# Eight plain products in the second pair too, and more identity products ahead of the first data

## The chip, the cores and the metric

The program runs on one core of a Trainium2 chip. The metric is the device time in microseconds (us) of one execution; less is better. TensorE is called PE here, VectorE DVE, ScalarE ACT, GpSimd POOL, and SyncE SP, as in the profile.

## The reference

```python
kv = np.einsum('bhsd,bhse->bhde', k, v)          # batch 4, heads 8, seq 576, head dim 64
out = np.einsum('bhsd,bhde->bhse', q, kv)
rms = np.sqrt(np.mean(out * out, axis=-1, keepdims=True) + 1e-06)
x = out / rms * g_norm                            # then heads side by side: x is 2304 x 512
h = x @ w_in                                      # 512 x 2048
x = (h * (1.0 / (1.0 + np.exp(-h)))) @ w_out      # 2048 x 512
y = ((x @ w_a) * (x @ w_b)) @ w_out2              # 512 x 1536 twice, 1536 x 512
```

All of it is float32.

## The kernel before

The tokens are worked on in two groups of 1152 (two batches each). Group 0's attention stands first, alone; then come four segments: layer 1 of group 0, layer 1 of group 1, layer 2 of group 0, layer 2 of group 1. Group 1's attention is cut into small slots (`attend(at)`) that stand between the matmuls of layer 1.

A segment runs over **pairs**: a pair is 256 columns of the up weights. For a pair the kernel needs a 2 x 2 block product, (two halves of the 512 features) x (two halves of the tokens), and forms it from seven products instead of eight, by Strassen's method in Winograd's form: POOL makes sums of weight quarters, and once in a segment DVE and POOL make sums of the x quarters (s1 to s4, in `x_sums`). To keep float32 accuracy each operand is split in a high and a low part (`x_hi`, `x_lo`; `w_hi`, `w_lo`), and each product is 12 matmuls of 128x128 by 128x288 (hi*hi, hi*lo, lo*hi; two halves c of the contraction; two halves s of the tokens). A product of seven adds results: ACT copies a partial sum (`part`, into `kept`), DVE adds it (`add`). Then ACT makes the sigmoid, DVE multiplies (`silu`), ACT rounds g to its high part (`g_round`), DVE makes the low part (`g_rest`). For a plain product x itself is the operand, and no sum of x or of weights is wanted.

The **first pair** already uses eight plain products (table `PLAIN`, function `plain(k)` on PE, line 750), since the sums of x are not there yet. It is short of other work: its down products stand in the second pair. In the first pair of before DVE and POOL also make the sums of x for the second pair and split them: on DVE `half_sum` (line 1275), `last_sum` (1283) and `half_rest` (1290), on POOL `half_sum` (567) and `half_rest` (574). Operands are numbered: 0, 3, 6, 7 are quarters of x, 1, 2, 4, 5 are the sums. The **second pair** then uses the seven products in an order of its own (`SECOND_STEPS`), and between them stand the 16 down tiles of the first pair, 6 matmuls each (`down1`, lines 798 to 800), which DVE takes out of PSUM (`flush1`, line 1370) from two banks that the tiles and the attention slots use in turn.

Each engine has its own list of instructions, in the order in which the code calls them, and waits on semaphores: PE waits for `w_ready` (weights split by POOL into a ring of four), `x_ready` and `side_ready` (x split by DVE and POOL), `g_ready` (a result bank read out to the end), and `flushed`. The order is written out by hand in the functions `first_pair`, `second_pair` and `layer1` of each engine.

At the very start PE multiplies the identity by itself `WARM` = 9 times (line 898), then turns q of head pair 0 (`q_turn`, line 679), and then waits for k and v by DMA (`kv`, line 665; its eviction is `kv_keep` on ACT; `q_kv`, line 691, follows it; `o_turn`, line 701, turns the result).

Of the kernel before, what the change touches and what calls it, by code (L numbers as in the profile page):

```python
# [11 lines left out]
P = 128  # L12
# [3 lines left out]
def fused_attention_ffn_kernel(nc, q, k, v, g_norm, w_in, w_out, w_a, w_b, w_out2, out):  # L16
# [51 lines left out]
    FIRST_TILES = (0, 3, 1, 2)  # L68
    FIRST_ENDS = {0: 3, 3: 4, 1: 5, 2: 7}
    FIRST_BANK = {0: BANK_A, 1: BANK_C, 2: BANK_A, 3: BANK_B}  # L70

    SECOND_STEPS = (5, 3, 0, 1, 2, 4, 6)
# [4 lines left out]
    DVE_RESTS = (((3, 0), (6, 0), (3, 1), (6, 1), (2, 0), (2, 1), (1, 0), (1, 1), (4, 0), (4, 1)),  # L77
# [5 lines left out]
    WARM = 9  # L83

    with ExitStack() as ctx:
# [139 lines left out]
        def at_step(u, n):  # L225

            return SECOND_STEPS.index(n) if u == 1 else n

        def after(u, n):

            return len(PLAIN) + STEPS * (u - 1) + at_step(u, n) + 1

        def weight(u, n):

            return RING + STEPS * (u - 1) + at_step(u, n)

        def sums_before(u, per):

            return per * (u - 1)

        def g_count(pp, tile):

            return 4 * pp + (FIRST_TILES.index(tile) if pp == 0 else tile) + 1

        def place(pp, tile):
            if pp == 0:
                return both(FIRST_BANK[tile])
            return halves(held[:, 2, :]) if tile == 2 else both({0: BANK_B, 1: BANK_A, 3: BANK_C}[tile])
# [61 lines left out]
        for pp in range(PAIR0[-1] + 1):  # L310
            tiles = D_TILES[SEGS[seg_of(pp - 1)][1]] if pp else 0
            steps = STEPS if pp < PAIR0[1] else 0
            for n in range(steps):
                slot_turn.append(turns)
                at = STEPS * pp + n
                turns += SLOT_BANKS[at % SLOTS] if at < SLOTS * PAIRS else 0
                for _ in range(TILES_AFTER[n] if pp else 0):
                    tile_turn.append(turns)
                    turns += 1
# [23 lines left out]
        def x_summed(seg, n, c=1):  # L343

            if seg == 0:
                if n == 5:
                    return side_sum, c + 1
                at = {1: 1, 2: 2, 4: 3}[n]
                return (x_sum, at) if c else (side_sum, 2 + at)
# [14 lines left out]
        def temps(seg):  # L364

            if seg == 0:
                return [x_sums[:, n] for n in (2, 1, 4, 5)]
# [18 lines left out]
        def _(sp):  # L386
            def raw_free(r):
# [6 lines left out]
                elif r == 0:  # L394
                    sp.wait_ge(w_ready, RING)
# [66 lines left out]
        def _(pool):  # L462
# [6 lines left out]
            def ready(u, step, src):  # L469
                n = weight(u, step)  # L470

                pool.wait_ge(prod, (3, 5, 7, 8)[n - RING] if n < 2 * RING else n + 1)
# [42 lines left out]
            def second_up():  # L515
                b11, b12, b21, b22 = quarters(1)
                nc.gpsimd.tensor_tensor(t2, b22, b12, ALU.subtract).then_inc(w_sum, 1)
                pool.wait_ge(w_sum, 1)
                ready(1, 5, t2)
                ready(1, 3, b21)  # L520
                nc.gpsimd.tensor_tensor(t0, b12, b11, ALU.subtract).then_inc(w_sum, 1)
                ready(1, 0, b11)
                pool.wait_ge(w_sum, 2)
                nc.gpsimd.tensor_tensor(t1, b22, t0, ALU.subtract).then_inc(w_sum, 1)
                pool.wait_ge(w_sum, 3)
                ready(1, 1, t1)
                ready(1, 2, t0)
                ready(1, 4, b22)
                pool.wait_ge(w_ready, weight(1, 2) + 1)
                nc.gpsimd.tensor_tensor(t0, b21, t1, ALU.subtract).then_inc(w_sum, 1)  # L530
                pool.wait_ge(w_sum, 4)
                ready(1, 6, t0)

            def head_pairs():
# [103 lines left out]
            second_up()  # L638
            lower(1)
# [6 lines left out]
        def _(pe):  # L646
# [91 lines left out]

            def plain(k):

                n, w, bank, begins = PLAIN[k]
                pe.wait_ge(w_ready, w + 1)
                at = PLAIN_SLOT[w]
                for c in range(2):
                    pe.wait_ge(*x_split(0, n, c))
                    hi, lo = w_hi[:, at, c, :], w_lo[:, at, c, :]
                    for w_part, x, first, last in ((hi, x_hi, c == 0, False), (hi, x_lo, False, False),
                                                   (lo, x_hi, False, c == 1)):
                        for s in range(2):
                            mm = pe.matmul(ps[:, bank + s, 0:PART], w_part,  # L750
                                           x[:, x_place(n), c, s * PART:(s + 1) * PART],
                                           start=(begins and first), stop=last, skip_group_check=not begins)
                mm.then_inc(prod, 1)

            def may_begin(u, n):
# [4 lines left out]
                if u == 1 and n in (1, 2, 4, 5):  # L760
# [4 lines left out]
                if n in STEP_BEGINS:  # L765
# [6 lines left out]
                    else:  # L772
                        tile = ({0: 2, 3: 3, 5: 1} if pp == 1 else {0: 1, 3: 0, 5: 3})[n]
# [12 lines left out]
            def down1(pp, n):  # L786
# [4 lines left out]
                pe.wait_ge(g_ready, g_count(pp, (1, 2)[m] if pp == 0 else 2 * m + 1))  # L791
# [54 lines left out]

            def layer1(pp):
# [759 lines left out]
```

## Time and profile before

| | |
|---|---|
| median of 3 runs | 897.32 us (896.08 to 897.57) |
| profiled execution | 897.5 us, of which the span of the profile is 895.7 |
| PE busy | 868.0 us (97%) |
| weight loads of PE (PEld) | 821.9 us (92%) |
| DVE, ACT, POOL busy | 520.8, 282.0, 626.3 us |

PE is nearly always busy after the start, so the share of PE's idle time by stretch, and the places where it waits, are what there is to read. "PEclk" is the clock that the throttle granted.

### The profile page before, as it was taken

To read this page: it belongs to the slowest core of one execution; us is meant where nothing else is said; L and a number is where in the kernel's file an instruction comes from. 1 tells how busy PE (TensorE), PEld (TensorE's weight loads), DVE (VectorE), ACT (ScalarE), POOL (GpSimd) and SP (SyncE) were. 2 spreads that over 40 slices of the span, in tenths; PEclk is the share of its full clock that TensorE was granted. 3 is DMA by queue.
4 is the path that set the end of the run, shared out by engine and by line. 5 is a ranking of instruction groups with operands and counts; after the bars stand their busy time and mean duration, and the time that the engine had idled before them with its cause. 6 is when DMAs were issued, how large, how long until landed. Compare 5 with 4: busy or idle time off the path is not lost.

```text
span 895.7 us, 16996 instructions
## 1 busy us (share of the span) xinstructions
PE 868.0 (97%) x6582; PEld 821.9 (92%) x6582; DVE 520.8 (58%) x816; ACT 282.0 (31%) x470; POOL 626.3 (70%) x911
## 2 busy tenths in 40 slices
PE   7889999999999999999999999999999999999998
PEld 6678899999999999999989999999998999999996
DVE  2697575657887665556774454453573544545536
ACT  2764353434543322222432121121251221211210
POOL 1596446654597777775588687887979877777760
PEclk9999999999999999999999999999999999999999
DMA  9742232510011111111111011111110250111103
GB/s 269 177 101 75 67 62 56 120 47 26 27 45 48 48 49 48 49 48 48 33 40 48 25 48 50 46 48 48 48 48 25 84 140 24 52 48 44 48 25 106
DMA packets 47103, 55.63 MB, mean 62 GB/s; under 512 B 11952, under 2 KB 32432, under 8 KB 47024
## 3 DMA queue, kind: packets, MB, share of 16 engines
q1 hardware_dynamic: 44304, 49.55, 20.1%
q10 hardware_dynamic: 2720, 4.98, 1.9%
q8 instruction: 54, 0.88, 0.4%
q14 instruction: 25, 0.20, 0.1%
HBM read 49.81 MB, written 4.72 MB: 61 GB/s over the span
## 4 chain that ended last, share of the span: by engine, by line
PE 86%; DVE 7%; POOL 2%; issue 2%; ACT 1%; DMA 1%; SPq 0%; DVEq 0%; ACTq 0%; POOLq 0%
PE ps L734 45%; PE ps L798 7%; PE ps L799 7%; PE ps L800 7%; PE ps L820 5%; PE ps L822 5%; PE ps L821 5%; PE ps L691 2%; DVE x_lo L1290 2%; DMA kvq<-in_v_dram 1%; PE ps L665 1%; PE ps L701 1%; DVE g_lo L1358 1%; DVE o_sb L1249 1%; DVE ps L1336 1%
## 5 line engine op out<-in xcount | busy, mean ns | idle before, releaser
L734 PE MATMUL ps<-x_hi,w_hi 128*128 128x288 f32 x1092 | 236.5, 298 | 4.8 <-ACT kept L1038 2.4
L734 PE MATMUL ps<-x_lo,w_hi 128*128 128x288 f32 x1092 | 234.0, 296 | 0.0
L734 PE MATMUL ps<-x_hi,w_lo 128*128 128x288 f32 x1092 | 232.9, 295 | 0.0
L734 PEld LDWEIGHTS ps<-x_hi,w_hi 128*128 128x128 f32 x1092 | 179.1, 188 | 17.1 <-POOL w_lo L478 5.0
L734 PEld LDWEIGHTS ps<-x_hi,w_lo 128*128 128x128 f32 x1092 | 176.1, 189 | 0.0
L734 PEld LDWEIGHTS ps<-x_lo,w_hi 128*128 128x128 f32 x1092 | 174.7, 188 | 0.0
L476 POOL TENSOR_SCALAR w_hi<-wt 128x256 fp32r<-128x256 f32 x156 | 70.4, 451 | 129.4 <-PE ps L734 125.1
L798 PE MATMUL ps<-g_hi,d_hi 128*128 128x288 f32 x512 | 154.2, 301 | 3.2 <-DVE g_lo L1358 1.2
L1038 ACT COPY kept<-ps 128x576 f32<-128x576 f32 x117 | 75.1, 642 | 254.2 <-PE ps L734 253.4
L1372 DVE TENSOR_TENSOR xy<-xy,ps 128x288 f32<-128x288 f32 x224 | 100.8, 453 | 88.5 <-PE ps L800 87.5
L800 PE MATMUL ps<-g_hi,d_lo 128*128 128x288 f32 x512 | 150.9, 295 | 0.0
L799 PE MATMUL ps<-g_lo,d_hi 128*128 128x288 f32 x512 | 150.9, 295 | 0.0
L478 POOL TENSOR_TENSOR w_lo<-wt,w_hi 128x256 fp32r<-128x256 f32 x156 | 117.6, 754 | 13.0
L1382 DVE TENSOR_TENSOR xy<-xy,ps 128x512 f32<-128x512 f32 x90 | 61.6, 685 | 95.1 <-PE ps L822 95.1
L798 PEld LDWEIGHTS ps<-g_hi,d_hi 128*128 128x128 f32 x512 | 96.4, 188 | 6.9 <-issue 3.2
L478 POOL TENSOR_TENSOR w_lo<-raw,w_hi 128x256 fp32r<-128x256 f32 x121 | 90.1, 745 | 10.1
L476 POOL TENSOR_SCALAR w_hi<-raw 128x256 fp32r<-128x256 f32 x121 | 51.4, 425 | 65.1 <-PE ps L734 65.1
L800 PEld LDWEIGHTS ps<-g_hi,d_lo 128*128 128x128 f32 x512 | 96.1, 188 | 0.0
L799 PEld LDWEIGHTS ps<-g_lo,d_hi 128*128 128x128 f32 x512 | 96.1, 188 | 0.0
L1063 ACT CAST g_hi<-ps 128x576 fp32r<-128x576 f32 x85 | 54.5, 642 | 102.7 <-DVE ps L1347 52.2
L820 PE MATMUL ps<-d_hi,g_hi 128*128 128x512 f32 x216 | 85.2, 395 | 0.0
L822 PE MATMUL ps<-d_hi,g_lo 128*128 128x512 f32 x216 | 84.7, 392 | 0.0
(104 smaller groups left out, 1211.4 us busy)
## 6 DMA issues: line engine op xcount, KB each, us to landing
raw<-in_moe_w_out_dram SPq DMA_DIRECT2D x28, 512.0 KB, 3.8
raw<-in_moe_w_in_dram SPq DMA_DIRECT2D x15, 512.0 KB, 3.5
raw<-in_moe_w_a_dram SPq DMA_DIRECT2D x12, 512.0 KB, 3.6
raw<-in_moe_w_b_dram SPq DMA_DIRECT2D x12, 512.0 KB, 3.5
kvq<-in_k_dram SPq DMA_DIRECT2D x12, 288.0 KB, 5.1
kvq<-in_v_dram SPq DMA_DIRECT2D x12, 288.0 KB, 6.6
out_dram<-xy SPq DMA_DIRECT2D x27, 128.0 KB, 2.4
kvq<-in_q_dram SPq DMA_DIRECT2D x16, 144.0 KB, 6.4
```

What stands on the lines that cost most here:

```text
L476: nc.gpsimd.tensor_scalar(w_hi[:, slot], src, 1.0, 0.0, ALU.mult, ALU.add).then_inc(w_high, 1)
L478: nc.gpsimd.tensor_tensor(w_lo[:, slot], src, w_hi[:, slot].bitcast(F32), ALU.subtract).then_inc(w_ready, 1)
L734: mm = pe.matmul(ps[:, bank + s, 0:PART], w, x[:, n, c, s * PART:(s + 1) * PART], start=(begins and first), stop=last, skip_group_check=no ...
L798: pe.matmul(dst, hi, g_hi[:, f, part], start=(f == 0), stop=False)
L799: pe.matmul(dst, hi, g_lo[:, f, part], start=False, stop=False)
L800: mm = pe.matmul(dst, lo, g_hi[:, f, part], start=False, stop=(f == 1))
L820: pe.matmul(dst, hi, d_hi[:, pp % 2, f, :], start=(f == 0), stop=False)
L822: mm = pe.matmul(dst, lo, d_hi[:, pp % 2, f, :], start=False, stop=(f == 1))
L1038: nc.scalar.copy(halves(kept[:, n, :]), both(BANK_A)).then_inc(part_kept, 1)
L1063: nc.scalar.copy(halves(g_at_half(g_hi, pp, m, f)), src).then_inc(g_high, 1)
L1372: nc.vector.tensor_tensor(dst, dst, src, ALU.add).then_inc(flushed, 1)
L1382: nc.vector.tensor_tensor(dst, dst, src, ALU.add).then_inc(flushed, 1)
```

## The change

The second pair is given eight plain products too, from the same quarters of x, and the same weight quarters of its own columns. So POOL makes four weight splits for it instead of four sums and seven splits, ACT no partial copies and DVE no adds. The sums of x and their splits, which stood in the first pair, are made in the second pair (operand 4's split in the third), for the third pair, which is now the first with seven products. `lower(0)` (the split of the first down weights) stands on POOL ahead of the sums of x. The sum s4 gets a place of its own, in `held`. At the start PE has 12 identity products ahead of the turns of q and 13 more behind them, instead of 9 and none.

```diff
-    PLAIN = ((0, 0, BANK_A, True), (0, 1, BANK_C, True), (7, 0, BANK_B, True), (3, 2, BANK_A, False),
-             (6, 2, BANK_B, False), (3, 3, BANK_C, False), (7, 1, BANK_A, True), (6, 3, BANK_A, False))
+    PLAIN = (((0, 0, BANK_A, True), (0, 1, BANK_C, True), (7, 0, BANK_B, True), (3, 2, BANK_A, False),
+              (6, 2, BANK_B, False), (3, 3, BANK_C, False), (7, 1, BANK_A, True), (6, 3, BANK_A, False)),
+             ((0, 0, BANK_B, True), (3, 2, BANK_B, False), (0, 1, BANK_C, True), (3, 3, BANK_C, False),
+              (7, 0, BANK_A, True), (6, 2, BANK_A, False), (7, 1, BANK_B, True), (6, 3, BANK_B, False)))
-    SECOND_STEPS = (5, 3, 0, 1, 2, 4, 6)
+    PLAIN_PAIRS = 2
+    PLAIN_TILES_AFTER = 2
-    WARM = 9
+    WARM = (12, 13)
...
@@ POOL
             def second_up():
-                ...            (four sums of weight quarters, seven splits)
+                quarter = quarters(1)
+                def second_split(at):
+                    w = PLAIN_SLOT.index(at)
+                    pool.wait_ge(prod, after(0, max(k for k in range(8) if PLAIN[0][k][1] == w)))
+                    split(RING + at, at, quarter[w])
+                second_split(0)
+                second_split(1)
+                half_sum(5, 0)
+                half_sum(5, 1)
+                second_split(2)
+                second_split(3)
+                half_sum(1, 0)
+                half_sum(2, 0)
             def head_pairs():
...
-                half_sum(5, 0)
-                half_sum(5, 1)
-                half_sum(1, 0)
-                half_sum(2, 0)
-                half_rest(5, 0)
-                half_rest(5, 1)
             head_pairs()
             lower(0)
             second_up()
+            half_rest(5, 0)
+            half_rest(5, 1)
             lower(1)
@@ PE
+            def second_pair():
+                t = 0
+                for k in range(len(PLAIN[1])):
+                    if PLAIN[1][k][3]:
+                        pe.wait_ge(g_ready, (g_count(0, 3), g_count(0, 1), g_count(0, 2), g_count(1, 0))[k // 2])
+                    plain_half(1, k, 0)
+                    if k < STEPS:
+                        attend(STEPS + k)
+                    plain_half(1, k, 1)
+                    for _ in range(PLAIN_TILES_AFTER):
+                        down1(0, t)
+                        t += 1
-            for _ in range(WARM):
-                pe.matmul(ps[:, BANK_D, 0:P], ident[:], ident[:], start=True, stop=True)
+            warm(WARM[0])
             for j in range(JS):
                 q_turn(0, 0, j, first_bank(0, j))
+            warm(WARM[1])
             kv(0, 0)
@@ ACT
             def first_pair():
...
-                first_round(5)
-                first_round(1)
                 sigmoid(0, 0)
                 attend(1, True)
-                first_round(2)
                 g_round(0, 0)
...
             def second_pair():
+                at = STEPS
+                attend(at, False)
+                sigmoid(1, 0)
+                attend(at + 2, True)
+                first_round(5)
+                g_round(1, 0)
+                attend(at + 3, True)
+                first_round(1)
+                sigmoid(1, 1)
+                attend(at + 4, True)
+                g_round(1, 1)
+                first_round(2)
+                attend(at + 5, True)
...
@@ DVE
             def first_pair():
...
                 half_rest(3, 1)
-                half_sum(1)
                 half_rest(6, 1)
-                half_sum(2)
                 silu(0, 0)
-                half_rest(2, 0)
                 g_rest(0, 0)
...
             def second_pair():
+                half_sum(1)
                 flush(0, 1)
                 norm(at + 1)
-                flush(2, 4)
+                flush(2, 3)
+                last_sum()
                 norm(at + 2)
+                silu(1, 0)
...
```

On PE, at the start of the program, the list is this before (`ident` is the identity, `q_tiles` are q's tiles, `kvq` holds k and v of a head pair):

```order
L898 MATMUL ps<-ident 128x128 x9
L679 MATMUL ps<-ident,q_tiles_53 128x128 x9
L665 MATMUL ps<-kvq_71 64x64 x36
L691 MATMUL ps<-kv_sb,qT_sb 64x128 x18
L665 MATMUL ps<-kvq_72 64x64 x36
L679 MATMUL ps<-ident,q_tiles_54 128x128 x9
```

and this in the change:

```order
L917 MATMUL ps<-ident 128x128 x12
L678 MATMUL ps<-ident,q_tiles_53 128x128 x9
L917 MATMUL ps<-ident 128x128 x13
L664 MATMUL ps<-kvq_71 64x64 x36
L690 MATMUL ps<-kv_sb,qT_sb 64x128 x18
L664 MATMUL ps<-kvq_72 64x64 x36
L678 MATMUL ps<-ident,q_tiles_54 128x128 x9
```

Thirteen products stand between the turns of q and the first product of k and v.

On DVE, in the first pair, from the last normalised tiles of the attention on, before:

```order
L1249 TENSOR_TENSOR o_sb<-ps,stat 128x384 x3
L1290 TENSOR_TENSOR x_lo<-xy,x_hi 128x576 x3
L1275 TENSOR_TENSOR x_sums<-xy,x_sums 128x576
L1290 TENSOR_TENSOR x_lo<-xy,x_hi 128x576
L1275 TENSOR_TENSOR x_sums<-xy 128x576
L1336 TENSOR_TENSOR ps<-held,ps 128x2x288
L1290 TENSOR_TENSOR x_lo<-x_sums,x_hi 128x576
L1358 TENSOR_TENSOR g_lo<-ps,g_hi 128x576
```

and in the change:

```order
L1268 TENSOR_TENSOR o_sb<-ps,stat 128x384 x3
L1308 TENSOR_TENSOR x_lo<-xy,x_hi 128x576 x4
L1354 TENSOR_TENSOR ps<-held,ps 128x2x288
L1376 TENSOR_TENSOR g_lo<-ps,g_hi 128x576
L1354 TENSOR_TENSOR ps<-held,ps 128x2x288
```

The two sums (`x_sums`) and the split of a sum are gone from between x's splits and the first `silu` and `g_rest`.

On DVE again, in the second pair of the change, from the first sum on, the flushes are the `COPY xy<-ps` rows:

```order
L1294 TENSOR_TENSOR x_sums<-xy,x_sums 128x576
L1388 COPY xy<-ps 128x288 x2
L1254 RECIPROCAL stat<-stat 128x18
L1268 TENSOR_TENSOR o_sb<-o_sb,stat 128x384
L1388 COPY xy<-ps 128x288 x2
L1301 TENSOR_TENSOR held<-xy,x_sums 128x1152
L1268 TENSOR_TENSOR o_sb<-o_sb,stat 128x384
L1354 TENSOR_TENSOR ps<-held,ps 128x2x288
L1388 COPY xy<-ps 128x288 x2
L1376 TENSOR_TENSOR g_lo<-ps,g_hi 128x576
L1294 TENSOR_TENSOR x_sums<-xy 128x576
```

The sums now stand between the flushes of the down tiles.

## Rows read from the trace of the kernel before

**Rows 1.** The page: busy time (share, instructions); and one group, its mean in ns.

```profile
PE 868.0 (97%) x6582; PEld 821.9 (92%) x6582; DVE 520.8 (58%) x816; ACT 282.0 (31%) x470; POOL 626.3 (70%) x911
...
L1063 ACT CAST g_hi<-ps 128x576 fp32r<-128x576 f32 x85 | 54.5, 642 | 102.7 <-DVE ps L1347 52.2
```

**Rows 2.** Busy time by stretch: us, then PE, PEld, DVE, ACT, POOL, clock, DMA share, GB/s.

```profile
65.50:96.00 30.50, 28.22 (x268) 26.61 (x265) 22.30 (x35) 13.65 (x25) 18.95 (x26) 1.00 0.27 65
```

**Rows 3.** Timeline of PE, 0 to 27 us: start, duration, what, count [idle before, releaser].

```profile
1.56 4.21 PE L898 MATMUL ps<-ident 128*128 128x128 f32 x18 [1.56 <-POOL ident L466]
6.86 2.18 PE L679 MATMUL ps<-ident,q_tiles 128*128 128x128 f32 x9 [1.09 <-POOL q_tiles L582]
11.91 2.20 PE L665 MATMUL ps<-kvq 64*64 64x64 f32 x72 [2.86 <-DMA kvq<-in_v_dram]
15.13 4.11 PE L691 MATMUL ps<-kv_sb,qT_sb 128*64 128x128 f32 x36 [1.02 <-issue]
19.16 2.09 PE L665 MATMUL ps<-kvq 64*64 64x64 f32 x72
21.18 1.20 PE L679 MATMUL ps<-ident,q_tiles 128*128 128x128 f32 x9
...
23.39 0.88 PE L691 MATMUL ps<-kv_sb,qT_sb 128*64 128x128 f32 x12
...
26.76 1.28 PE L665 MATMUL ps<-kvq 64*64 64x64 f32 x72
```

**Rows 4.** Timeline of POOL, the copies of q's tiles of head pairs 0 to 2.

```profile
6.30 1.40 POOL L582 COPY q_tiles<-kvq 128x384 f32<-128x384 f32 x3 [4.79 <-DMA kvq<-in_q_dram]
18.09 1.41 POOL L582 COPY q_tiles<-kvq 128x384 f32<-128x384 f32 x3 [10.39 <-DMA kvq<-in_q_dram]
24.26 1.41 POOL L582 COPY q_tiles<-kvq 128x384 f32<-128x384 f32 x3 [4.76 <-DMA kvq<-in_q_dram]
```

**Rows 5.** Timeline of PE in the first pair and at its end.

```profile
52.23 0.43 PE L750 MATMUL ps<-x_hi,w_lo 128*128 128x288 f32 x2
54.27 0.53 PE L750 MATMUL ps<-x_hi,w_hi 128*128 128x288 f32 x2 [1.60 <-DVE x_lo L1290]
...
57.09 0.49 PE L679 MATMUL ps<-ident,kvq 128*128 128x128 f32 x3
59.75 0.53 PE L750 MATMUL ps<-x_hi,w_hi 128*128 128x288 f32 x2 [2.17 <-DVE g_lo L1358]
...
65.57 0.53 PE L734 MATMUL ps<-x_hi,w_hi 128*128 128x288 f32 x2
```

**Rows 6.** Timeline of DVE in the first pair, and one later split of x.

```profile
44.62 5.81 DVE L1290 TENSOR_TENSOR x_lo<-xy,x_hi 128x576 fp32r<-128x576 f32 x3
...
54.13 1.98 DVE L1275 TENSOR_TENSOR x_sums<-xy 128x576 f32<-128x576 f32 x1
...
57.34 1.69 DVE L1290 TENSOR_TENSOR x_lo<-x_sums,x_hi 128x576 fp32r<-128x576 f32 x1 [0.55 <-ACT x_hi L1025]
...
75.85 0.75 DVE L1290 TENSOR_TENSOR x_lo<-x_sums,x_hi 128x576 fp32r<-128x576 f32 x1
```

**Rows 7.** Timeline of POOL, the first sums of x, and the second pair.

```profile
44.59 3.32 POOL L567 TENSOR_TENSOR x_sums<-xy 128x576 f32<-128x576 f32 x2
...
77.07 0.41 POOL L476 TENSOR_SCALAR w_hi<-wt 128x256 fp32r<-128x256 f32 x1 [3.05 <-PE ps L734]
```

**Rows 8.** Groups of DVE by form, 65.5 to 96.1 us: count, busy us, mean ns, idle before.

```profile
L1370 DVE COPY xy<-ps 128x288 f32<-128x288 f32 x14 | 6.0, 451 | 4.2 <-PE ps L800 4.2
L1290 DVE TENSOR_TENSOR x_lo<-x_sums,x_hi 128x576 fp32r<-128x576 f32 x4 | 4.6, 1179 | 0.0
...
L1336 DVE TENSOR_TENSOR ps<-held,ps 128x576 f32<-128x576 f32 x3 | 2.3, 755 | 0.4 <-ACT held L1050 0.4
L1283 DVE TENSOR_TENSOR x_sums<-xy,x_sums 128x1152 f32<-128x1152 f32 x1 | 1.8, 1791 | 0.0
```

**Rows 9.** Timeline of PE, the first matmuls of the third pair.

```profile
96.04 0.42 PE L734 MATMUL ps<-x_hi,w_hi 128*128 128x288 f32 x2
```

More of the change, by code:

```diff
@@ L315, in fused_attention_ffn_kernel @@
                 at = STEPS * pp + n
-                turns += SLOT_BANKS[at % SLOTS] if at < SLOTS * PAIRS else 0
-                for _ in range(TILES_AFTER[n] if pp else 0):
+                turns += SLOT_BANKS[at % SLOTS] if n < STEPS and at < SLOTS * PAIRS else 0
+                for _ in range(0 if pp == 0 else PLAIN_TILES_AFTER if pp == 1 else TILES_AFTER[n]):
                     tile_turn.append(turns)
@@ L393, in raw_free @@
                     sp.wait_ge(d_ready, 2 * (PAIR0[n] + p + 1))
-                elif r == 0:
-                    sp.wait_ge(w_ready, RING)
+                elif p < PLAIN_PAIRS and n == 0:
+                    sp.wait_ge(w_ready, RING * (p + 1))
                 else:
@@ L737, in half, with plain_half @@
                     mm.then_inc(prod, 1)
-            def plain(k):
[L741 to L753, printed above, removed]
+            def plain_half(pp, k, c):
+                n, w, bank, begins = PLAIN[pp][k]
+                at = PLAIN_SLOT[w]
+                if c == 0:
+                    pe.wait_ge(w_ready, w + 1 if pp == 0 else RING + at + 1)
+                if pp == 0:
+                    pe.wait_ge(*x_split(0, n, c))
+                hi, lo = w_hi[:, at, c, :], w_lo[:, at, c, :]
+                for w_part, x, first, last in ((hi, x_hi, c == 0, False), (hi, x_lo, False, False),
+                                               (lo, x_hi, False, c == 1)):
+                    for s in range(2):
+                        mm = pe.matmul(ps[:, bank + s, 0:PART], w_part,
+                                       x[:, x_place(n), c, s * PART:(s + 1) * PART],
+                                       start=(begins and first), stop=last, skip_group_check=not begins)
+                if c == 1:
+                    mm.then_inc(prod, 1)
+            def plain(k):
+                plain_half(0, k, 0)
+                plain_half(0, k, 1)
             def may_begin(u, n):
@@ L894, in layer2, with warm @@
                 down2(pp - 1, 8)
+            def warm(count):
+                for _ in range(count):
+                    pe.matmul(ps[:, BANK_D, 0:P], ident[:], ident[:], start=True, stop=True)
             pe.wait_ge(consts, 3)
-            for _ in range(WARM):
-                pe.matmul(ps[:, BANK_D, 0:P], ident[:], ident[:], start=True, stop=True)
+            warm(WARM[0])
             for j in range(JS):
                 q_turn(0, 0, j, first_bank(0, j))
+            warm(WARM[1])
             kv(0, 0)
@@ L919, in _ @@
             first_pair()
-            for pp in range(1, PAIR0[-1]):
+            second_pair()
+            for pp in range(PLAIN_PAIRS, PAIR0[-1]):
                 if SEGS[seg_of(pp)][1] == 1:
@@ L1022, in first_round @@
                 if n == 4:
-                    act.wait_ge(prod, 7)
+                    act.wait_ge(prod, after(1, 6))
                 nc.scalar.copy(x_hi[:, n], operand(0, n)).then_inc(x_high, 1)
@@ L1041, in sigmoid @@
                 u, idx = prods_of(pp)[0], g_count(pp, tile) - 1
-                if pp == 0:
-                    act.wait_ge(prod, FIRST_ENDS[tile] + 1)
+                if pp < PLAIN_PAIRS:
+                    act.wait_ge(prod, after(pp, PLAIN_ENDS[pp][tile]))
                 elif tile == 1:
@@ L1414, in flush @@
                         flush1(0, n)
+                half_sum(1)
                 flush(0, 1)
                 norm(at + 1)
-                flush(2, 4)
+                flush(2, 3)
+                last_sum()
                 norm(at + 2)
-                half_rest(4, 0)
-                flush(5, 7)
+                silu(1, 0)
+                dve.wait_ge(*x_summed(0, 4))
+                flush(4, 5)
+                g_rest(1, 0)
+                half_sum(2)
                 norm(at + 3)
-                half_rest(4, 1)
-                add(u, 0, both(BANK_B))
+                flush(6, 7)
+                silu(1, 1)
+                dve.wait_ge(*x_summed(0, 2, 0))
+                dve.wait_ge(*x_summed(0, 2))
                 flush(8, 9)
-                add(u, 1, halves(held[:, 2, :]))
+                g_rest(1, 1)
+                half_rest(1, 0)
                 flush(10, 11)
-                silu(1, 0)
-                g_rest(1, 0)
+                half_rest(1, 1)
+                silu(1, 3)
                 flush(12, 13)
-                silu(1, 1)
-                g_rest(1, 1)
+                g_rest(1, 3)
+                half_rest(2, 0)
+                flush(14, 15)
                 silu(1, 2)
-                add(u, 2, both(BANK_C))
-                flush(14, 15)
+                half_rest(2, 1)
                 g_rest(1, 2)
-                silu(1, 3)
-                g_rest(1, 3)
             def layer1(pp):
@@ L1452, in layer1 @@
                 late_rest(pp, 0)
+                if pp == 2:
+                    half_rest(4, 0)
                 if pp == 7:
@@ L1458, in layer1 @@
                 late_rest(pp, 1)
+                if pp == 2:
+                    half_rest(4, 1)
                 next_rest(pp, 0)
```

98 lines of the change are left out of this document (31 added, 67 removed).

## The prediction

> **What bounds the kernel now.** I read the page first. PE is busy 868.0 of 895.7 us [rows 1], so what can be won is the rest, and any product added costs its full time unless it fills a hole. So I asked for PE's timeline and looked for places where its starts stand further apart than its matmuls need. They lie almost all in the first 100 us, in three parts.
>
> *The start.* PE multiplies the identity until 5.8 us, waits for q's tiles, turns them, and then stands from 9 to 11.9 us waiting for v by DMA [rows 3]. The reader is to see that the same work costs two prices there: nine turns take 2.18 us at 6.86 and 1.20 us at 21.18; 72 records of k and v take 2.20 us at 11.91, 2.09 us at 19.16, and 1.28 us at 26.76; twelve records of `q_kv` take 0.88 us at 23.39, and 36 take 4.11 us at 15.13 [rows 3]. That is PE's lower level, 1.2 GHz, up to about 21.1 us, and 2.4 GHz from there on. The column of the granted clock doesn't show it (it reads 1.00 in every stretch I asked for); the distances do: eight gaps between nine turns, less one tail, are (2.18 - 0.42)/8 = 0.22 us and later (1.20 - 0.15)/8 = 0.13 us. Ahead of the rise PE had worked without a real pause from 15.13 us, 6 us; the identity products of before are one stretch of 3.9 us, after which it stood 1.1 us.
>
> *The first pair.* PE's starts at 52.23 and 54.27 are two matmuls (0.27 us) apart by count, so 1.77 us are lost, to DVE's `x_lo`. Three turns from 57.09 need 0.35 us, and the next start is 59.75: 2.31 us lost, to `g_lo` [rows 5]. Both come from DVE's list [rows 6]: three splits of x take 5.81 us together, a sum 1.98 us, a split 1.69 us, while later one split of the same shape takes 0.75 us. In the slow stretch POOL is working on x as well (two sums in 3.32 us [rows 7]).
>
> *The second pair.* From 65.57 [rows 5] to 96.04 [rows 9] are 30.47 us. A step of product is 12 matmuls, and six issues of two stand 0.265 us apart, 1.59 us; seven are 11.1 us. A down tile is 6 matmuls, 0.79 us; 16 are 12.7. The slots of the attention in it (three `o_turn` at a third of a us, one `kv` at 1.28 less its tail, one `q_turn`) come to 2.5 us. That is 26.3 us, so 4.2 us are lost. By busy time it is less, 30.50 - 28.22 = 2.3 us [rows 2], since the ends are modelled and cover part of each hole; I go by starts.
>
> **The change, part by part.**
>
> *Identity products.* 12 are 24 records at 0.22 us (18 took 4.21 us, less a tail of 0.42, over 17 gaps [rows 3]), 5.3 us, from 1.56 to 6.85. The turns of q could start at 6.86 before, POOL's copy being the limit (6.30 us [rows 4]), and still can: this part costs nothing, and its cover is that copy; without it it would cost 1.3 us (six records more). Then 13 more, 26 records: at the lower level 5.6 us, from 8.7 to 14.3, which is 2.4 us past the arrival of v at 11.9; at the upper level half, 2.8 us, done at 11.5 and hidden by that DMA. Which holds is decided by whether the clock is up by then. Now PE works from 1.56 on without a pause over 0.2 us, 7 us by the time the 13 begin, and 6 us was what stood ahead of the rise before. I take it that the clock is up. The Trainium skill (TensorE: Matmul & The Clock Gate, Part 1) says that the throttled state is the default and activity releases it; the prices above agree.
>
> Then `kv` takes 0.8 us less (2.09 against 1.28), `q_kv` of head 0 takes 3 x 0.81 = 2.4 us instead of 4.03: PE would be at the second `kv` at 16.75 instead of 19.16, and through it at 18.0. But q of head pair 1 lands at 18.09, and PE follows the copy by 0.56 us (6.30 to 6.86 [rows 3, 4]): its turns start at 18.65 instead of 21.18. That is 2.5 us, and the DMA caps it. The next, 24.26 + 0.56 = 24.8, is before PE's shifted time (about 25.4), so nothing takes it back. ACT, DVE and POOL follow PE in this part. **Term: -2.5 us**; bounds: 0 (clock not up, where the 2.4 us of delay are about paid back by the work behind it at full clock), and -2.9.
>
> *First pair.* DVE has the fourth split of x right behind the third. POOL works on `lower(0)` beside it, so I leave the slow price: 44.62 + 4 x 1.94 = 52.4 us at the latest, where PE asks at 52.5. So the 1.77 us go. `silu(0,0)` follows at once (0.76), `g_round` on ACT takes 0.64 [rows 1, 8], `g_rest` 0.76: with hand-overs of 0.1 us, ready at 54.6 to 54.9. PE comes there after two products less the hole, at 55.5. The 2.31 us go too, with 0.6 us to spare. What is late next would be `g_rest(0, 1)`, behind ACT's square of the first `q_kv`; by the same prices it is done near 59.7, and its tile is wanted at 62.8. **Term: -4.1 us**; bounds -3.2 and -4.3 (with the slower first matmul after each wait).
>
> *Second pair.* One product more: **+1.6 us**, on PE's own time, hidden by nothing. Three `part`, three `add`, four weight sums and three weight splits less; those were off the path (POOL stood 3.05 us waiting for PE at one split alone [rows 7]). The four splits of the second pair wait for the first pair's products 3, 5, 7 and 8 and are done some 0.5 to 7 us before they are wanted. What can cost is DVE: its list now has sums and splits between the flushes, and a flush that is late holds one of two banks, and so PE. Its work there: 16 flushes at 0.45, four `silu` and four `g_rest` at 0.76, six halves of x at 1.18, one whole sum 1.79, three normalised tiles at about 1.0 (a SBUF-only form like `x_lo`, two thirds as long): 7.2 + 6.1 + 7.1 + 1.8 + 3.0 = 25.2 us [rows 8], in 27.9 us of PE's work. Stepping through the list by these prices I get waits of about 0.3 us at the third turn, 0.5 us at the tile behind `kv` (it waits for ACT's eviction, before as now), and a few tenths at the end; I take 1.5 us for what I can't place, so the 4.2 become 1.5: **-2.7 us**. Bounds: 0.7 left, and all 4.2 left.
>
> The Trainium skill (SBUF — State Buffer, SBUF: two separate sides) speaks against this part: the port pair of DVE and POOL is an exclusive lock for a DVE operation with two SBUF inputs against a POOL operation that reads SBUF, and the loser waits for the whole instruction. The trace agrees: 1.94 us in the slow stretch, 0.75 us with POOL idle. By that rule alone, each of the six halves in the second pair would be at 1.98 us, and DVE's work at 30.0 us, more than PE's 27.9. It would hold only if POOL were always busy.
>
> *Third pair.* It takes `half_rest(4, c)`, and ACT's rounding of operand 4 (1.2 us) ahead of an eviction that PE's bank waits for. It had waits of the same size at this place. I count 0, bounds 0 and +1.0. Everything behind is PE's own pace as before.
>
> **Sum.** -2.5 - 4.1 + 1.6 - 2.7 = -7.7 us. The profiled execution is 897.5 us (895.7 and 1.8 around it), 0.2 us from the median of 897.3, so 889.8 from the one and 889.6 from the other; I say 889.6.
>
> **The rivals.**
>
> *The clock isn't up, or the 13 products run past 11.9 us.* For it: where the clock rose before, real data was being multiplied; half of the new stretch is turns. Then the first term is 0: 892.1, and 891 to 893.5. Chance 0.19.
>
> *DVE is the bound of the second pair.* DVE's work at the slow price is 30.0 us, with the restarts about 31: the second pair lasts 31 instead of my 29.4, and 0.5 us more in the third: 891.7. Against: POOL waits for PE in much of it. Chance 0.13.
>
> *Slower.* The ten operations of DVE on SBUF alone (six halves, one whole sum, three normalised tiles) each hold a flush. Two banks give a flush 0.79 us before PE stands, so an operation of 1.98 us can cost 1.2 us; ten are 12 us. Then the second pair is 27.9 + 12 = 39.9 us against 30.5, +9.4, and with -6.6 of the other terms the kernel ends at 900.1. It decides from about 0.9 us each (8.4 us in all, for +1.8). Against: in the second pair of before four splits and one whole sum stood between the flushes too [rows 8], and all its waits together were 4.2 us. Chance 0.04.
>
> *The work is only moved.* All that the first pair gains is paid back in the third, which now wants the sums: 897.3 - 2.5 + 1.6 = 896.4. Against: the sums have 25 us more. Chance 0.03.
>
> *Better:* all holes go and the kernel is under 887.5. Chance 0.07. **The forecast** has 0.54, in 887.6 to 891.2.
>
> **The numbers.** A measurement tells 0.2% (1.8 us) from no change. Faster: 0.54 + 0.19 + 0.13 + 0.07 = 0.93; same 0.03; slower 0.04. The range leaves out the slower case, the moved case and the edges of the others: 887.0 to 893.2.
>
> **What would show it.** In the profile after: turns of q at 6.86 and nine of them in 1.2 to 2.2 us; the 13 products end before 11.9 us; `q_kv` 36 records in about 2.5 us; the second head's turns at 18.65. No wait for `x_lo` or `g_lo` over 0.3 us in the first pair; second pair begins near 59.0 and ends near 88.4, with PE's waits for `xy` (flush) as the sign of DVE's part. The prediction is wrong if the 13 products are over 0.4 us each, or if DVE has no idle time in the second pair.

## The result, and the profile after

The changed kernel takes 895.09 us (median of 20 runs, 893.36 to 896.98), the kernel before 897.79 us on the same chips (20 runs, 895.17 to 899.60). The ratio is 0.9974, with a 95% interval from 0.9965 to 0.9984: faster by 2.7 us, or 0.3%, where 7.7 us were forecast. The profiled execution is 895.0 us (span 893.2), against 897.5 us (span 895.7) before. Three stretches tell the story: up to the third pair, from there to 240 us, and around 674 us.

**Up to the third pair** the kernel did more than was forecast. The timeline of PE at the start answers to [rows 3]:

```profile
1.57 4.65 PE L917 MATMUL ps<-ident 128*128 128x128 f32 x24 [1.57 <-POOL ident L469]
6.75 1.45 PE L678 MATMUL ps<-ident,q_tiles 128*128 128x128 f32 x9 [0.53 <-POOL q_tiles L579]
8.03 3.07 PE L917 MATMUL ps<-ident 128*128 128x128 f32 x26
11.63 1.28 PE L664 MATMUL ps<-kvq 64*64 64x64 f32 x72 [0.53 <-DMA kvq<-in_v_dram]
13.94 2.19 PE L690 MATMUL ps<-kv_sb,qT_sb 128*64 128x128 f32 x36 [1.03 <-issue]
...
18.55 0.50 PE L664 MATMUL ps<-kvq 64*64 64x64 f32 x18 [1.32 <-issue]
19.11 1.45 PE L678 MATMUL ps<-ident,q_tiles 128*128 128x128 f32 x9
...
38.28 0.53 PE L750 MATMUL ps<-x_hi,w_hi 128*128 128x288 f32 x2
...
58.13 0.53 PE L750 MATMUL ps<-x_hi,w_hi 128*128 128x288 f32 x2
...
86.81 0.42 PE L733 MATMUL ps<-x_hi,w_hi 128*128 128x288 f32 x2
```

The 13 products behind the turns end at 11.1 us, ahead of v at 11.63, and `kv` takes 1.28 us and `q_kv` 2.19, both the upper level's prices, where before they took 2.20 and 4.11. The last three rows are the first plain product of the first pair, the start of the second pair, and the start of the third. They stood at 41.35, 65.57 [rows 5] and 96.04 [rows 9] before. So PE leads by 3.07, 7.44 and 9.23 us, and the second pair takes 28.68 us instead of 30.47.

POOL's copy of q for the second head pair, which answers to the second of [rows 4], is held by the DMA:

```profile
18.55 1.41 POOL L579 COPY q_tiles<-kvq 128x384 f32<-128x384 f32 x3 [10.96 <-DMA kvq<-in_q_dram]
```

The timeline of DVE, which answers to [rows 6]:

```profile
41.55 1.96 DVE L1308 TENSOR_TENSOR x_lo<-xy,x_hi 128x576 fp32r<-128x576 f32 x2
44.06 2.90 DVE L1308 TENSOR_TENSOR x_lo<-xy,x_hi 128x576 fp32r<-128x576 f32 x2 [0.54 <-ACT x_hi L1039]
...
50.61 0.76 DVE L1376 TENSOR_TENSOR g_lo<-ps,g_hi 128x576 fp32r<-128x576 f32 x1 [0.70 <-ACT g_hi L1087]
```

All four splits of x are done at 46.96 us, and the first `g_lo` at 51.37, where PE asks for it at 52.33. PE waits for neither any more. In the second pair DVE's operations by form are these (count, busy us, mean ns, idle before):

```profile
L1388 DVE COPY xy<-ps 128x288 f32<-128x288 f32 x15 | 6.7, 454 | 7.5 <-PE ps L805 7.5
...
L1376 DVE TENSOR_TENSOR g_lo<-ps,g_hi 128x576 fp32r<-128x576 f32 x4 | 3.0, 750 | 0.4 <-ACT g_hi L1087 0.4
L1308 DVE TENSOR_TENSOR x_lo<-x_sums,x_hi 128x576 fp32r<-128x576 f32 x3 | 2.5, 827 | 0.0
```

The flushes wait 7.5 us for PE's tiles, and in PE's waits of this pair none is for a flush: DVE is never the later one. Three of the splits have a mean of 827 ns, where [rows 8] had 1179.

**From the third pair to about 240 us** the lead melts. Here is the same work in both: a stretch of the kernel before (first fence), and one that holds nearly the same instructions after (second). The columns are those of [rows 2].

```profile
98.00:240.00 142.00, 139.30 (x1210) 134.26 (x1209) 89.41 (x162) 61.39 (x108) 77.59 (x115) 1.00 0.26 63
```

```profile
89.00:236.00 147.00, 142.63 (x1207) 134.24 (x1206) 90.90 (x162) 61.90 (x109) 77.70 (x116) 1.00 0.25 61
58.10:86.80 28.70, 28.61 (x278) 28.06 (x277) 20.63 (x35) 15.06 (x25) 17.20 (x19) 1.00 0.38 85
```

1210 and 1207 matmuls, 134.2 us of weight loads in both, a granted clock of 1.00 in both, and yet 5.0 us more. The second row of the second fence is the second pair, where PE is busy 28.61 of 28.70 us. By PE's starts the lead is still 9.1 us at the first turn of the fourth pair (127.47 us before, 118.33 after). From there it shrinks by a few tenths at a time to 4.3 us at the tile behind the last attention slot (239.35 and 235.09), and then it stays. What PE waits for in the longer stretch is seen in the chain of its weight loads and its matmuls (total us, times, longest). Before:

```profile
PE ps L798 <- ACT qT_sb L978: 0.6, 1, 0.6
...
PEld ps L798 <- issue: 1.4, 3, 0.8
```

After:

```profile
PE ps L803 <- ACT qT_sb L1002: 1.1, 2, 0.7
PE ps L803 <- ACT xy L982: 0.5, 1, 0.5
PE ps L803 <- ACT o_sb L969: 0.2, 1, 0.2
...
PEld ps L803 <- issue: 4.5, 15, 0.7
```

L803 is the first matmul of a down tile, and what it waits for on ACT are evictions of the attention: turned q (`qT_sb`), the output (`o_sb`), and the output turned (`xy`). Fifteen times a weight load of a down tile comes late, against three before. The profile names nothing that these wait for ("issue"); that the banks are behind them too is shown by e1 and e2 below. One such place, PE's timeline before:

```profile
148.16 0.49 PE L679 MATMUL ps<-ident,kvq 128*128 128x128 f32 x3
...
149.01 0.43 PE L734 MATMUL ps<-x_hi,w_lo 128*128 128x288 f32 x2
149.28 0.29 PE L798 MATMUL ps<-g_hi,d_hi 128*128 128x288 f32 x1
```

and after:

```profile
139.26 0.52 PE L678 MATMUL ps<-ident,kvq 128*128 128x128 f32 x3
...
140.15 0.43 PE L733 MATMUL ps<-x_hi,w_lo 128*128 128x288 f32 x2
140.98 0.37 PE L803 MATMUL ps<-g_hi,d_hi 128*128 128x288 f32 x1 [0.41 <-ACT qT_sb L1002]
```

The order is the same: a turn of q, half a product, a down tile. The tile now stands 0.83 us behind the last start instead of 0.27, because it waits for the turn's eviction. A tile has to wait for the eviction of the turn just ahead of it only if both use one bank.

**Around 674 us** the last loss stands, of another kind. The timeline of PE after:

```profile
673.93 0.65 PE L733 MATMUL ps<-x_hi,w_hi 128*128 128x288 f32 x2 [1.89 <-POOL w_lo L481]
674.38 0.68 PE L733 MATMUL ps<-x_lo,w_hi 128*128 128x288 f32 x2
...
677.26 0.59 PE L733 MATMUL ps<-x_lo,w_hi 128*128 128x288 f32 x2
677.68 0.42 PE L733 MATMUL ps<-x_hi,w_lo 128*128 128x288 f32 x2
```

the row of its stretch, where the third number from the end is the granted clock:

```profile
675.00:680.00 5.00, 5.00 (x27) 4.79 (x26) 0.76 (x1) 0.64 (x1) 4.75 (x9) 0.74 0.30 100
```

and the timeline of the same place before:

```profile
678.13 0.53 PE L734 MATMUL ps<-x_hi,w_hi 128*128 128x288 f32 x2 [1.87 <-POOL w_lo L478]
```

Both kernels stand 1.9 us there, for POOL's split of a weight at the first pair of the last segment. In this execution of the changed kernel the granted clock went down behind it (0.74 as a mean of 675 to 680 us, the issues of two matmuls 0.48 us apart instead of 0.265, which is 1.2 against 2.4 GHz). Eight distances from 673.93 to 677.68 are 3.75 us instead of 2.1, so 1.6 us are lost.

The three add up: 9.2 us of lead at the third pair, less 5.0, less 1.6, is 2.6; the spans differ by 2.5.

### The profile page after: what moved, and what is told of

Same layout as the page of the kernel before. It is cut to its first block, busy times and chain, and to the rows that moved or that the text cites. A ratio compares the mean times of both kernels' runs of the same rounds, so it can differ in the third digit from the quotient of the medians.

```text
span 893.2 us, 17059 instructions
## 1 busy us (share of the span) xinstructions
PE 872.3 (98%) x6626; PEld 824.4 (92%) x6626; DVE 512.3 (57%) x813; ACT 279.9 (31%) x467; POOL 618.0 (69%) x901
## 4 chain that ended last, share of the span: by engine, by line
PE 89%; DVE 4%; POOL 2%; issue 2%; DMA 1%; ACT 1%; SPq 1%; DVEq 0%; ACTq 0%; POOLq 0%
PE ps L733 44%; PE ps L803 8%; PE ps L805 7%; PE ps L804 7%; PE ps L825 5%; PE ps L827 5%; PE ps L826 5%; PE ps L750 3%; PE ps L690 2%; DMA kvq<-in_q_dram 1%; PE ps L700 1%; PE ps L664 1%; POOL w_lo L481 1%; PE ps L678 1%; DVE ps L1354 0%
## 5 line engine op out<-in xcount | busy, mean ns | idle before, releaser
L733 PE MATMUL ps<-x_hi,w_hi 128*128 128x288 f32 x1064 | 230.5, 298 | 5.0 <-ACT kept L1062 2.3
L733 PE MATMUL ps<-x_lo,w_hi 128*128 128x288 f32 x1064 | 228.7, 297 | 0.0
L733 PE MATMUL ps<-x_hi,w_lo 128*128 128x288 f32 x1064 | 227.4, 295 | 0.0
L733 PEld LDWEIGHTS ps<-x_hi,w_hi 128*128 128x128 f32 x1064 | 175.2, 189 | 17.2 <-issue 5.0
L733 PEld LDWEIGHTS ps<-x_hi,w_lo 128*128 128x128 f32 x1064 | 172.2, 189 | 0.0
L733 PEld LDWEIGHTS ps<-x_lo,w_hi 128*128 128x128 f32 x1064 | 171.0, 189 | 0.0
L803 PE MATMUL ps<-g_hi,d_hi 128*128 128x288 f32 x512 | 155.1, 303 | 2.9 <-ACT qT_sb L1002 1.1
L1062 ACT COPY kept<-ps 128x576 f32<-128x576 f32 x114 | 73.2, 642 | 253.0 <-PE ps L733 252.2
L481 POOL TENSOR_TENSOR w_lo<-wt,w_hi 128x256 fp32r<-128x256 f32 x152 | 114.1, 751 | 12.7
L803 PEld LDWEIGHTS ps<-g_hi,d_hi 128*128 128x128 f32 x512 | 96.4, 188 | 8.5 <-issue 5.8
L805 PEld LDWEIGHTS ps<-g_hi,d_lo 128*128 128x128 f32 x512 | 96.1, 188 | 0.0
L804 PEld LDWEIGHTS ps<-g_lo,d_hi 128*128 128x128 f32 x512 | 96.1, 188 | 0.0
```

Source lines behind the costliest of these rows:

```text
L481: nc.gpsimd.tensor_tensor(w_lo[:, slot], src, w_hi[:, slot].bitcast(F32), ALU.subtract).then_inc(w_ready, 1)
L733: mm = pe.matmul(ps[:, bank + s, 0:PART], w, x[:, n, c, s * PART:(s + 1) * PART], start=(begins and first), stop=last, skip_group_check=no ...
L803: pe.matmul(dst, hi, g_hi[:, f, part], start=(f == 0), stop=False)
L804: pe.matmul(dst, hi, g_lo[:, f, part], start=False, stop=False)
L805: mm = pe.matmul(dst, lo, g_hi[:, f, part], start=False, stop=(f == 1))
L1062: nc.scalar.copy(halves(kept[:, n, :]), both(BANK_A)).then_inc(part_kept, 1)
```

## The experiments

**Where the two banks part.** The down tiles and the attention's one-bank slots share two banks, `BANK_D + turn % 2`; `tile_turn` and `slot_turn` hold each one's number in the common order. Part of the diff that the section on the change leaves out is the loop that numbers them:

```diff
-            steps = STEPS if pp < PAIR0[1] else 0
+            steps = len(PLAIN[0]) if pp == 1 else STEPS if pp < PAIR0[1] else 0
             for n in range(steps):
                 slot_turn.append(turns)
                 at = STEPS * pp + n
-                turns += SLOT_BANKS[at % SLOTS] if at < SLOTS * PAIRS else 0
+                turns += SLOT_BANKS[at % SLOTS] if n < STEPS and at < SLOTS * PAIRS else 0
```

The second pair has eight steps and seven slots. The count of turns has its guard (`n < STEPS`), the append has none. So `slot_turn` gets an entry at index 14 that belongs to no slot. Slot 14 reads it (28 instead of 30, the same bank), and each slot from 15 on reads the turn of the slot ahead of it. Worked out from the loop: slot 15 should have turn 33, between tiles with 32 and 34; it reads 30, and all three have the same bank. Of the 26 slots with one bank from 14 on, 17 land on the bank of the tiles on both sides (the expectation below says 16); none did before. PE and ACT read the same table, so they meet in one bank as ever; only the alternation with the tiles is lost.

*e1_own_turns* gives the slots their own turns again:

```diff
             for n in range(steps):
-                slot_turn.append(turns)
+                if n < STEPS:
+                    slot_turn.append(turns)
```

> The change, with the eighth step of the second pair no longer adding an entry to the table of slot turns, so that every attention slot from the third pair on has its own turn of the two PSUM banks again. All arithmetic is the same. Theory A (turns): in the change 16 of the 26 one-bank slots behind the second pair share a bank with the tile ahead and the tile behind, and PE waits there; the lead of 9.5 us that the change has at 98 us melts to 4.3 us by 230 us for that alone. Then this kernel keeps it: 4.5 to 5.5 us under the change, near 890, and PE's small waits at the down tiles between 89 and 236 us are gone. Rival B (moved work): DVE and ACT are late in the third to eighth pair because the sums and roundings stand later; then this kernel is within 0.5 us of the change.

Measured: 889.57 us (4 runs, 888.24 to 890.00), against 897.31 (17 runs) for the kernel before; ratio 0.9905, interval 0.9887 to 0.9923. The medians are 7.7 us apart, which is the sum that was forecast; the interval of the ratio allows 6.9 to 10.1 us. Here is the row of the same stretch in e1 (columns as above):

```profile
90.00:232.00 142.00, 139.20 (x1209) 134.17 (x1208) 90.39 (x163) 62.13 (x109) 77.51 (x115) 1.00 0.26 63
```

The late weight loads of its down tiles:

```profile
PEld ps L804 <- issue: 0.6, 2, 0.3
```

And PE's timeline:

```profile
140.13 0.49 PE L679 MATMUL ps<-ident,kvq 128*128 128x128 f32 x3
...
140.98 0.43 PE L734 MATMUL ps<-x_hi,w_lo 128*128 128x288 f32 x2
141.25 0.29 PE L804 MATMUL ps<-g_hi,d_hi 128*128 128x288 f32 x1
```

142.0 us as before, 0.27 us between the last start and the tile's, two late weight loads instead of fifteen. And the lead no longer melts. These are PE's starts at the same places in the three traces, and the lead over the kernel before:

| place | before | changed kernel | lead | e1 | lead |
|---|---|---|---|---|---|
| third pair, first product | 96.04 | 86.81 | 9.2 | 88.34 | 7.7 |
| fourth pair, first turn of the output | 127.47 | 118.33 | 9.1 | 119.40 | 8.1 |
| fifth pair, last `q_kv` | 164.47 | 156.99 | 7.5 | 156.44 | 8.0 |
| sixth pair, last turn of q | 200.13 | 193.28 | 6.9 | 192.09 | 8.0 |
| seventh pair, last slot | 231.90 | 226.81 | 5.1 | 223.86 | 8.0 |
| a down tile behind it | 239.35 | 235.09 | 4.3 | 231.37 | 8.0 |

*e2_before_late_turns* puts the same fault into the kernel before, and nothing else of the change, right behind the loop:

```diff
+        slot_turn.insert(14, slot_turn[14])
```

> The kernel before, with one entry more in its table of slot turns at slot 14, so that slots from the third pair on use the turn of the slot ahead of them; nothing else is changed. Theory A: 4 to 5.5 us slower than the kernel before (near 902.5), lost between 100 and 240 us. Rival B: within 0.5 us of the kernel before.

Measured: 902.41 us (6 runs, 900.55 to 904.23), ratio 1.0054, interval 1.0038 to 1.0070: +5.1 us. PE's waits from 98 to 246 us in e2 show the picture of after:

```profile
PEld ps L800 <- issue: 5.4, 16, 0.8
```

and in the timeline the same tile as above waits:

```profile
150.48 0.37 PE L800 MATMUL ps<-g_hi,d_hi 128*128 128x288 f32 x1 [0.41 <-ACT qT_sb L980]
```

Taken away from the change, the shift gives 5.0 us if each kernel is set against the kernel before that was measured with it (-2.7 and -7.7), and 5.5 by the medians themselves (895.09 to 889.57, not measured side by side); added to the kernel before, it costs 5.1. The cause is settled from both sides. That the second pair's work was merely paid back later, as the rival "only moved" had it, is ruled out: e1 moves the same work and keeps it all.

**What the parts are worth by themselves.** *e3_identity_only* is the kernel before with the identity products alone:

```diff
-    WARM = 9
+    WARM = (12, 13)
...
-            for _ in range(WARM):
+            for _ in range(WARM[0]):
...
+            for _ in range(WARM[1]):
+                pe.matmul(ps[:, BANK_D, 0:P], ident[:], ident[:], start=True, stop=True)
```

> The kernel before with 12 identity products ahead of the first turns of q and 13 behind them, as in the change; nothing else. By the traces of before and of the change the turns of head pair 1 start 2.1 us earlier and the second kv group of the first pair 3.0 us earlier: 2.5 to 3.2 us faster than before. Rival C: the gain is given back at the waits for x_lo and g_lo of the first pair, since DVE's list there is POOL-bound and POOL starts its work on a DMA that does not come earlier: under 1.5 us.

Measured: 894.90 us (12 runs, 893.14 to 896.71), ratio 0.9973, interval 0.9961 to 0.9984: -2.4 us. Its timeline has `kv` and `q_kv` at the upper level, and the two waits of the first pair, which were 1.60 and 2.17 us [rows 5], smaller, not larger:

```profile
11.80 1.28 PE L665 MATMUL ps<-kvq 64*64 64x64 f32 x72 [0.48 <-DMA kvq<-in_v_dram]
...
51.13 0.53 PE L750 MATMUL ps<-x_hi,w_hi 128*128 128x288 f32 x2 [1.12 <-DVE x_lo L1292]
...
55.68 0.53 PE L750 MATMUL ps<-x_hi,w_hi 128*128 128x288 f32 x2 [1.23 <-DVE g_lo L1360]
```

Time won ahead of the first pair is not eaten by its waits. At the second pair this trace leads by 3.9 us (61.69 against 65.57), and it loses 1.5 of them again to the granted clock behind the stand at 674 us (0.57 from 674 to 678 us).

*e4_pair_only* is the other half: own turns, and identity products as before (nine and none).

```diff
-    WARM = (12, 13)
+    WARM = (9, 0)
...
+                if n < STEPS:
```

> The kernel with own turns, and the 9 identity products of before (none behind the turns of q): the pair part of the change alone, without the turn slip. Theory A with additive parts: the full lead less that of the identity products, 6 to 6.7 us faster than before, 2.5 to 3.2 us slower than the kernel with own turns.

Measured: 892.32 us (6 runs, 891.48 to 895.07), ratio 0.9943, interval 0.9928 to 0.9958: -5.0 us, where the terms of the two pairs were -4.1 + 1.6 - 2.7 = -5.2. The two parts are -7.4 together and e1 is -7.7: they add up.

**Which identity products hold the clock.** *e6_first_twelve* has the twelve ahead and none behind, *e7_behind_only* nine ahead and the thirteen behind, both with own turns.

```diff
-    WARM = (12, 13)
+    WARM = (12, 0)          (e6_first_twelve)
+    WARM = (9, 13)          (e7_behind_only)
```

> The kernel with own turns, with 12 identity products ahead of the turns of q and none behind. Theory A (the 13 behind hold the clock while PE would wait for v): PE idles from about 8 to 11.6 us, the first kv and q_kv groups are at the lower level again in most runs, and the kernel is 2 to 3 us slower than with own turns, like the one with 9 and none. Rival B (the three more ahead raise the clock and it stays up): within 0.6 us of the kernel with own turns.

> The kernel with own turns, with 9 identity products ahead and 13 behind the turns of q. Theory A (those behind do it): within 0.8 us of the kernel with own turns. Rival B (the clock is not up in time, the 13 run past the arrival of v at half speed): 1 to 2.5 us slower than with own turns.

Measured: e6 892.45 us (5 runs, 891.04 to 893.12), ratio 0.9950, interval 0.9936 to 0.9964; e7 889.16 us (12 runs, 886.90 to 896.28), ratio 0.9940, interval 0.9918 to 0.9962 (kernel before 897.00, 17 runs). The median of e7 lies 7.8 us under that of the kernel before, its ratio stands for 5.4, since five of its twelve runs are 3 us or more above the others. PE's timeline in e6:

```profile
6.99 1.44 PE L679 MATMUL ps<-ident,q_tiles 128*128 128x128 f32 x9
11.99 2.20 PE L665 MATMUL ps<-kvq 64*64 64x64 f32 x72 [3.56 <-DMA kvq<-in_v_dram]
15.22 4.11 PE L691 MATMUL ps<-kv_sb,qT_sb 128*64 128x128 f32 x36 [1.03 <-issue]
```

and in e7:

```profile
6.79 1.44 PE L679 MATMUL ps<-ident,q_tiles 128*128 128x128 f32 x9 [1.43 <-POOL q_tiles L580]
8.07 3.07 PE L918 MATMUL ps<-ident 128*128 128x128 f32 x26
11.07 1.28 PE L665 MATMUL ps<-kvq 64*64 64x64 f32 x72
```

In e6 the turns have the short time (1.44 us), PE then stands 3.56 us for v, and `kv` and `q_kv` are back at 2.20 and 4.11 us. So the thirteen bridge the wait for v, and with it hold the clock. The traces of e2 and e4, with nine ahead and none behind, say the same: their turns have the short time (1.44 and 1.45 us), PE then stands 3.24 and 3.43 us for v, and `kv` is at 2.20 us. Nine ahead are enough in the profiled run of e7, which is the shortest of all, 886.9 us. Part of that is not the edit's: the DMA brings v and q at other times in each execution (`kv` starts at 11.07 us in e7 and 11.59 in e1, the second turns of q at 18.15 and 19.36). But the medians of e7 and e1 don't differ, and e7 spreads over 9 us: seven of its runs are between 886.9 and 889.3 us, and five, with a mean clock of 0.998 or 0.996, between 892.3 and 896.3. All four of e1 are within 1.8 us. The five have no profile, so that in them the clock wasn't up by `kv` is likely, and not shown; four runs of e1 are few to set against twelve.

**The wait at 674 us.** *e5_tile_ahead* has own turns, and at the first pair of the last segment puts a down tile of the pair before ahead of the step whose weight is late, not behind it:

```diff
+                if pp == PAIR0[3]:
+                    down2(pp - 1, 2)
...
-                down2(pp - 1, 2)
+                if pp != PAIR0[3]:
+                    down2(pp - 1, 2)
```

> The kernel with own turns, and in the first pair of the last segment (near 665 us) PE takes the third down tile ahead of step 3 instead of behind step 4. There PE waits 1.9 us for POOL's split of a weight in every profile, and in the profiles of the change and of the kernels with identity products only and with the pair part only the granted clock fell to half for 3.4 us right behind that wait. Theory A (the wait brings the fall of the clock): the tile (1.4 us) fills most of the wait, the clock no longer falls there in any run, and the kernel is 1.4 us plus the share of falls (0.8 us on average) better, about 2 us under the kernel with own turns, near 887.5. Rival B: the tile's time is only moved and the fall stays: 0 to 1.4 us better, with clocks of 0.998 as often as before.

Measured: 888.17 us (4 runs, 888.11 to 889.64), ratio 0.9912 to the kernel before at 897.00, interval 0.9899 to 0.9925. PE's waits from 600 to 700 us:

```profile
PE ps L734 <- issue: 1.1, 1, 1.1
PE ps L734 <- POOL w_lo L482: 0.5, 1, 0.5
```

against this in e1:

```profile
PE ps L734 <- POOL w_lo L482: 1.9, 1, 1.9
```

A tile takes up 1.4 us of the wait, but a pause of PE's own issue of 1.1 us has come up in the same stretch. The trace of e5 is 0.13 us behind that of e1 at 657 us, and 0.14 behind it at 679.6: the tile and the pause cancel. Three of the four runs have a mean clock of 1.00, at 888.1 to 888.2; the fourth is the profiled one, whose clock fell at the start (near 21 us), not at this place. The best run of e1, with a clock of 1.00 too, is 888.24. So the tile itself gave next to nothing. What the median has over e1's (1.4 us) could be a fall of the clock that doesn't come, but in e1's profiled run the fall is at 21 us and not here. With four runs each, not side by side, and intervals that overlap, that stays open. It is the best version that was made, 8.8 us under the kernel before.

## Why the prediction was wrong, step by step

The median lies 1.9 us above the top of the range, and 5.5 above the forecast. With the slots' own turns (e1) it would have been 889.6.

**The step that failed** is the last sentence of the part on the third pair: "Everything behind is PE's own pace as before." It puts everything behind the third pair at 0. The third pair itself kept to its 0: PE's lead is 9.2 us at its start and 9.1 at the start of the fourth. From the fourth pair to the end of the attention slots in the seventh it cost 4.9 us in the trace, and 5.0 to 5.5 in runs (e1, e2). The order of the instructions there is as before, and it was read for that; the banks that they use are not in the order, but in a table worked out by a loop, and the diff changes that loop. The numbers of that table for the slots behind the second pair would have shown it. The price can be read at the one place shown above: a tile on the same bank as the turn ahead of it starts 0.83 us behind the half product's last start instead of 0.27, about 0.56 us; nine such places would make 5 us, and there are 17, not all of which wait that long.

**Luck in the sum.** That the median of e1 is the forecast to a tenth is in part luck. The three terms were 1.5 us too small together: the changed kernel leads by 9.2 us at the third pair, not by 7.7. In e1's profiled run the clock takes most of that back at 20.6 to 24 us. The one run of e1 with a mean clock of 1.00 takes 888.24 us, 9.1 under the kernel before.

**The start (-2.5).** The mechanism is right: the clock was up for the thirteen products, and q of the second head pair capped the gain, as forecast, but at 18.55 us instead of 18.09. That the longer stretch ahead raises the clock is less sure: with nine ahead it was up for the turns in e2, e4 and e7 as well. What was needed were the thirteen, to hold it. The twelve took 4.65 us where 5.3 were reckoned, hidden behind q's copy either way. The term itself is 2.6 us in e3's trace (first plain product at 38.75 us against 41.35). That the medians have -2.4 is in part luck, as e3 wins another 1.4 us at the waits of the first pair and loses 1.5 at 674 us. In the changed kernel its turns stood at 19.11 instead of 18.65, so 2.07 us at this place. One more microsecond came ahead of the first pair: before, PE's own issue paused 1.26 us among the turns at 37.40; after, a pause of 1.32 us stands ahead of 18.55, where q was not there anyway. Nothing in the forecast said so; this microsecond is luck.

**The first pair (-4.1, bounds -3.2 and -4.3).** From its first plain product to the second pair it took 24.22 us (41.35 to 65.57) and takes 19.85: -4.4. Both waits are gone, a tenth outside the bound. I had left the splits of x at the slow price of 1.94 us; they took 0.98 and 1.45.

**The second pair (+1.6 - 2.7 = -1.1).** It is -1.8: 28.7 us, where 29.4 were forecast. Of the 1.5 us of waits that I took for what I couldn't place, 0.8 are left (28.7 less 27.9 of PE's work), and none is a wait for a flush. The rivals "DVE is the bound" (31 us) and "slower by its ten operations" are not borne out. The Trainium skill (SBUF — State Buffer, SBUF: two separate sides), which stood behind the first of them, would have the price of a split set by what POOL does at the time. The runs agree with it in direction: 1.94 us beside POOL's sums of x before, 1.45 beside its splits of down weights now, 0.98 beside its last split of w and first roundings of d, 0.75 later [rows 6]. The rival's 30.0 us of DVE's work take POOL as always at work; it was at work 17.2 of 28.7 us, and DVE's work was 20.6 us.

**The clock later on** was not in the forecast at all. The profiled run lost 1.6 us to it at 674 us. Over the 20 runs of the changed kernel those with a mean clock of 1.00 are at 893.4 to 893.9 us (8), with 0.998 at 895.0 to 895.9 (7), with 0.996 at 896.1 to 897.0 (5). So it moves single runs by 1.6 us or so, and it doesn't explain the miss: the best eight are still above the range. How much of it the kernel before has, its mean clocks (0.990 to 1.00 in 34 runs) don't tell. They are also low where the column has the lower level of the first 21 us in it: the profiled run of e4 (mean 0.992) reads 0.50 from 12 to 18 us, that of the kernel before (0.999) reads 1.00, at the same prices of `kv` and `q_kv`.

## What to carry to other kernels

When one loop is given another number of steps, print every table that it fills, of before and after, and compare not the order alone but the banks and buffers behind it, far behind the place that is meant to change. Where two users alternate between two banks, that alternation has a price: here 17 lost ones cost 5 us, two thirds of what the change brings without the fault, and the engines do the same work in the same order. And if a change gives less than its own stretch shows, align the two traces from their ends, and read where the lead melts.

## What was not expected of the hardware

- The granted clock can go down behind a short stand in the middle of steady work: 1.9 us of waiting at 672 us, then 1.2 GHz up to 677.3, and 1.6 us lost. It isn't certain to. Eight profiled runs stood 1.85 to 1.89 us at this place: behind it the column falls in those of the changed kernel, e2 (0.64 from 683.2 to 688 us), e3 and e4, and stays at 1.00 in those of the kernel before, e1, e6 and e7. What decides it, no run here tells.
- In e1 the clock was up from about 8 us on, PE stood 1.39 us for issue and 0.35 for q's copy between 17.1 and 19.4 us, and from 20.6 to 24 us it had the lower level (the first twelve of `q_kv` with 1.55 us instead of 0.88). Its row:

```profile
20.50:24.00 3.50, 3.27 (x21) 2.22 (x19) 2.33 (x6) 1.06 (x2) 0.26 (x1) 0.52 1.06 358
```

  In the profiled run of the changed kernel, with stands of 1.32 us there, it didn't fall. The third pair starts at 88.34 us in e1, 1.5 us behind the 86.81 of after; 0.25 of them stand at q's copy (19.36 against 19.11), the rest behind it.
- PE's own issue pauses 1.1 to 1.4 us at one place among the small matmuls of the attention, in the middle of a group for which the profile shows no wait, and at another place when the program ahead of it has another length: at 37.40 us before, 18.55 after, 17.70 in e7. What it is, no run here tells.
